# Third to eighth expert, last two tiles: two streams of one weight block joined into one of 512 columns, with VectorE adding the halves

## The reference, cut to what matters

```python
def _moe2_ref(x, w_gate, w_noise, noise, w1, w2):
    ...
    for e in range(E):                              # E = 8
        for k in range(2):
            mask = top2[:, k] == e
            h = np.maximum(x[mask] @ w1[e], 0.0)    # 512 -> 1024, the "up" product
            out[mask] += top2_w[mask, k, None] * (h @ w2[e])   # 1024 -> 512, "down"
```

## Time and profile before

| | us |
|---|---|
| median of three runs | 1014.07 (1013.69 to 1014.99) |
| the profiled execution | 1014.13 |
| its span, first to last instruction | 1012.3 |
| PE busy in it | 992.4 (98%) |
| DVE busy | 436.7 (43%) |
| ACT busy | 368.2 (36%) |
| POOL busy | 340.5 (34%) |

### The profile page before, as it was taken

How to read it: one execution, slowest core, us unless ns; L and a number is a source line. 1 busy time by engine, 2 the same in 40 slices (tenths; PEclk the granted TensorE clock), 3 DMA queues, 4 the chain that set the end, 5 groups by cost and what they waited for, 6 DMA issues and landing times. The chain is left out here.

```text
span 1012.3 us, 18602 instructions
## 1 busy us (share of the span) xinstructions
PE 992.4 (98%) x7173; PEld 903.5 (89%) x7173; DVE 436.7 (43%) x1188; ACT 368.2 (36%) x906; POOL 340.5 (34%) x317
## 2 busy tenths in 40 slices
PE   8999999999999999999999999999999999999994
PEld 7999898989989898999999898899998989898983
DVE  4664343442535345353355534443534434444410
ACT  5553343334324342432344423433434233343410
POOL 2780022121211212110112424563828373745211
PEclk9999999999999999999999999999999999999998
DMA  6655244242423324230234242772626465564312
GB/s 231 198 184 124 84 153 109 73 131 85 137 96 125 104 77 133 84 115 26 102 105 136 44 135 45 179 171 71 160 73 151 95 156 109 137 134 109 58 18 36
DMA packets 83098, 113.79 MB, mean 112 GB/s; under 512 B 19264, under 2 KB 45888, under 8 KB 83008
## 3 DMA queue, kind: packets, MB, share of 16 engines
q1 hardware_dynamic: 69104, 84.74, 27.8%
q0 software_dynamic: 13472, 27.31, 13.3%
q10 hardware_dynamic: 432, 0.52, 0.2%
HBM read 83.52 MB, written 29.02 MB: 111 GB/s over the span
## 5 line engine op out<-in xcount | busy, mean ns | idle before, releaser
L885 PEld LDWEIGHTS bank<-xr,wr 128*128 128x128 f32 x2592 | 325.0, 191 | 9.6 <-issue 0.8
L885 PE MATMUL bank<-xr,wr 128*128 128x256 f32 x2592 | 327.7, 283 | 0.4 <-issue 0.4
L986 PE MATMUL bank<-wr 128*128 128x256 f32 (+1 forms) x1536 | 229.3, 309 | 0.7 <-DVE xr L1554 0.4
L986 PEld LDWEIGHTS bank<-wr 128*128 128x128 f32 x1536 | 226.7, 190 | 2.2 <-DVE xr L1554 0.8
L707 POOL DMA_INDIRECT arena<-x_rows,shared x120 | 132.1, 1101 | 145.1 <-DVE v_nat L1542 96.8
L902 PE MATMUL bank<-wr,hr 128*128 128x512 f32 x648 | 174.9, 405 | 0.0
L1170 ACT ACTIVATE arena<-bank 128x256 f32<-128x256 f32 x108 | 41.4, 384 | 265.9 <-PE bank L885 257.0
L902 PEld LDWEIGHTS bank<-wr,hr 128*128 128x128 f32 x648 | 113.8, 188 | 26.9 <-issue 5.8
L1430 DVE SCALAR_TENSOR_TENSOR arena<-arena,bank 128x256 f32<-128x256 f32 x108 | 45.4, 420 | 211.6 <-ACT arena L1170 189.8
L1001 PE MATMUL bank<-wr 128*128 128x512 f32 x576 | 132.8, 390 | 0.0
L1001 PEld LDWEIGHTS bank<-wr 128*128 128x128 f32 x576 | 107.5, 188 | 21.9
(11 more groups left out here) (140 smaller groups left out, 739.9 us busy)
## 6 DMA issues: line engine op xcount, KB each, us to landing
arena<-moe_w SPq DMA_DIRECT2D x40, 512.0 KB
arena<-moe_w SPq DMA_DIRECT2D x96, 128.0 KB
p_rows<-arena SPq DMA_DIRECT2D x28, 256.0 KB, 2.1
v_nat<-p_rows SPq DMA_DIRECT2D x112, 64.0 KB
arena<-gv SPq DMA_DIRECT2D x12, 512.0 KB, 4.0
out<-zeros POOLq DMA_DIRECT2D x20, 256.0 KB, 3.2
x_rows<-arena SPq DMA_DIRECT2D x9, 512.0 KB, 4.3
arena<-v SPq DMA_DIRECT2D x34, 128.0 KB, 3.2
```

Source lines behind the costliest of these rows:

```text
L885: mm = pe.matmul(o, gv_w[:, f, w, kk], xr[:, g % 2, x, kk], start=(m + kk + n == 0), stop=(kk == KC - 1 and n == 2), skip_group_check=True)
L986: mm = pe.matmul(ps_h[u % 2][:, 0:n], w1_r[e % 2][:, a, kk, f * P:(f + 1) * P], xT[p][:, b, kk], start=(kk + x == 0), stop=(kk == KC - 1 a ...
```

## The change

For `p = 1` of experts 2 to 7 (`joint(e, p)`), a unit takes two matmuls for each `kk` in place of three. One has the high weights and streams the high and the low tokens one behind the other, 512 columns, into the two halves of the bank. The other has the low weights and streams the high tokens, 256 columns, into the first half. A new step on DVE, `add_hidden`, adds the two halves into `gate` with a `tensor_reduce` whose two inputs for each output lie 256 elements apart in the bank. `relu` and `hidden_low` of these units read `gate` instead of the bank. The new semaphore `hidden_added` tells ACT that the sum is there and PE that the bank is free; `joints(u)` counts the joined units up to `u`. Streamed columns of a unit stay as they were: 12 x 256 = 4 x 512 + 4 x 256 = 3072.

```diff
+        def joint(e, p):
+            return p == 1 and e >= AHEAD
+        def joints(u):
+            return sum(1 for i in range(u + 1) if i // F2C >= 2 * AHEAD and i // F2C % 2)
...
@@ up(e, p, f), on PE
-                if u >= 2:
+                if u >= 2 and joints(u - 2) > joints(u - 3):
+                    pe.wait_ge(hidden_added, joints(u - 2))
+                elif u >= 2:
                     pe.wait_ge(ht_lo, u - 1)
...
+                if joint(e, p):
+                    both = ps_h[u % 2].rearrange("p (a n) -> p a n", a=2)
+                    for kk in range(KC):
+                        pe.matmul(both, w1_r[e % 2][:, 0, kk, f * P:(f + 1) * P], xT[p][:, :, kk], start=(kk == 0), stop=False,
+                                  skip_group_check=True)
+                        mm = pe.matmul(both[:, 0], w1_r[e % 2][:, 1, kk, f * P:(f + 1) * P], xT[p][:, 0, kk], start=False,
+                                       stop=(kk == KC - 1), skip_group_check=True)
+                    mm.then_inc(up_done, 1)
+                    return
@@ relu(e, p, f), on ACT
+                if joint(e, p):
+                    act.wait_ge(hidden_added, joints(u))
+                    act.activation(hT[p][:, 0, f], gate[:, u % 2], ACT.Relu).then_inc(ht_hi, 1)
+                    return
@@ on DVE
+            def add_hidden(e, p, f):
+                u = F2C * half_no(e, p) + f
+                dve.wait_ge(up_done, u + 1)
+                dve.wait_ge(ht_lo, u - 1)
+                dve.tensor_reduce(gate[:, u % 2], ps_h[u % 2].rearrange("p (a n) -> p n a", a=2), AX.X, ALU.add
+                                  ).then_inc(hidden_added, 1)
...
@@ hidden_low(e, p, f)
+                if joint(e, p):
+                    dve.scalar_tensor_tensor(out=hT[p][:, 1, f], in0=gate[:, u % 2], scalar=0.0,
+                                             in1=hT[p][:, 0, f].bitcast(F32), op0=ALU.max, op1=ALU.subtract).then_inc(ht_lo, 1)
+                    return
```

More of the change, by code:

```diff
@@ L324, in attention_two_moe_program @@
         up_done = sem("up_done")
+        hidden_added = sem("hidden_added")
         ht_hi = sem("ht_hi")
@@ L1690, in _ @@
             for e in range(AHEAD, NE):
[L1691 to L1695, removed]
+                for f in range(F2C):
+                    hidden_low(e, 0, f)
+                    if f < KC:
+                        low(e, KC + f)
+                add_hidden(e, 1, 0)
+                for f in range(F2C):
+                    if f < F2C - 1:
+                        add_hidden(e, 1, f + 1)
+                    hidden_low(e, 1, f)
                 for a in range(TILES):
```

## The result

| | us |
|---|---|
| before, median of six runs | 1013.91 (1013.69 to 1014.99) |
| changed, median of six runs | 1019.25 (1017.47 to 1022.42) |
| ratio | 1.0052, 95% interval 1.0039 to 1.0065 |
| span of the profiled execution, before and after | 1012.3, 1018.2 |

The change is slower by half a per cent. 1011.5 us was forecast.

The account below looks back on a forecast made before the run. PE's matmul stream was taken to bound the kernel. Saving 53.3 ns in each of 48 units, 2.56 us, with nothing added by DVE or the later chain, gave 1011.5 us against 1014.07, range 1010.9 to 1014.3 us.

Parts of the forecast that it names:

- What bounds the kernel: Expert stretches of 55.40 us: PE busy throughout, so only the pace of its matmul stream counts.
- The fixed 13.3 ns for each matmul: Joined units: each matmul with weight load costs 13.3 ns beyond its columns; four fewer in each of 48 units save 2.56 us.
- rival (2): Joined units: the fixed 13.3 ns stays or switching widths costs as much, no gain, 1014.1 us; chance 0.13 with small gains.
- The reduction: DVE's `add_hidden`: reading 512 elements from the bank takes 0.69 us, whatever the distance between inputs.
- rival (1): DVE's `add_hidden`: far-apart inputs make the reduction slow, up to 1.22 us, PE waits, 1020.8 us; chance 0.12.
- The cover inside the joined part: Between joined units: PE's cover against waiting for the added halves grows from 0.40 to 0.50 us.
- The size of the delay: Behind the eighth unit: ACT's and DVE's work for the next expert starts 0.76 us later against PE.
- 384 matmuls fewer: Profile after the change: the count of matmuls was to fall by 384.
- the 2.5 ns: Skill page's gap for each warm matmul: by it only 0.5 us would go, giving 1013.6 us; the prediction followed the rows.
- What moves behind the units: Next expert's chain after the eighth unit: starting 0.76 us later costs nothing, with 6.7 us of room.
- Rival (3): Joined units: cover smaller than worked out, PE waits a little in some, 1012 to 1014 us; 0.05 with anything else.
- Slower: Outcome class for the whole kernel, slower than before: chance 0.14, from rival (1) and a remainder.

Follow-up runs that it names:

- b_late_084: Kernel before, plus a DVE operation of about 0.84 us ahead of the next expert's first transpose, experts 3 to 7, no joined matmuls: 1020.55 us, ratio 1.0057.
- a_unit_first: Changed kernel, with the fifth down tile and last tile's tokens handled on ACT and DVE only behind the next expert's first two up units: 1013.12 us, ratio 0.9986.
- b_late_short_low: Kernel before with the 0.84 us delay, and low parts of first-layer weight blocks of experts 4 to 8 cut to a quarter of their columns: 1014.65 us.
- a_short_low: Changed kernel, with low parts of first-layer weight blocks of experts 4 to 8 cut to a quarter of their columns: 1012.02 us, ratio 0.9977.

## Why the prediction was wrong, point by point

**Right.** What bounds the kernel: PE's stream. The fixed 13.3 ns for each matmul, in part: the joined parts shortened by 0.19 to 0.37 us where 0.43 was worked out, 1.50 us in place of 2.56 over the six. At 346 ns a pair the whole 13.3 ns that a pair was to save is gone; at 353 ns half of it is back, so rival (2) was half right in those parts. The reduction: 0.69 us forecast, 0.69 us measured, with inputs 256 elements apart in the bank, so rival (1) fell, and with it the worry that the rule of the Trainium skill ("SBUF — State Buffer", section "Door 1: The DMA port swizzle"), which is on matmuls, might hold for VectorE's reads of PSUM. The cover inside the joined part: no wait there in any trace. The size of the delay: "0.76 us later against PE"; the first transpose starts at 695.73 - 693.93 = 1.80 us after the first down matmul against 0.96 us before, so 0.84 us.

**Two slips that changed nothing.** "384 matmuls fewer" should be 192 (48 x 4; the profile's page counts 7173 before and 6981 after). And the 2.5 ns that the prediction takes from the section "Back-to-back issue gap" of the Trainium skill ("TensorE: Matmul & The Clock Gate") is given there for an isolated matmul, so it does not bear on a stream with weight loads like this one, whose 13.3 ns the rows give.

**The step that failed** is "What moves behind the units", with its "That costs nothing ... Cost nil, with 0.76 us of 6.7 us spent". It looked for the deadline of each moved piece at its own user: the third tile before the next p = 0 units (6.7 us of room), the last tile before the next p = 1 units (14 us). But the last tile has an earlier deadline that no user sets. In ACT's and DVE's queues the next expert's first `relu` and low part stand behind it, and PE needs these at its third unit. The row that gave the tile's end, 722.92 + 0.69 us, was read against 738.1 us; it had to be read against 725.62 us, less the `relu` and the low part that still have to follow. The cover there is 0.78 us. b_late_084 (the delay without the change costs 6.5 us) and a_unit_first (the late chain without that order costs nothing) show this step from both sides.

**A second miss in the same step** was to move the chain rigidly. The prediction names POOL's gathers among the late things, but gives them their old durations. Moved by 0.84 us, they fell over other DVE rows, took up to 0.77 us more each, and `rows_out` came 2.72 us later against PE. This miss was needed for the loss as well. In the kernel before ACT stands idle for 0.87 us ahead of that `relu`; with the last tile moved by 0.84 us and nothing lengthened, its low part would end at 722.92 + 0.69 + 0.84 = 724.45 us, 0.17 us after the moment at which the unit's low part starts now (724.28), and 0.6 us of the cover would be left. That is an estimate from these rows. It agrees with b_late_short_low and a_short_low, which show no break.

**A small miss**: the cover was worked out between joined units (0.50 us), not at the seam, where the second joined unit waits for a p = 0 unit's longer low part. It cost 0.055 us six times, 0.3 us in all.

Rival (3) named the right kind of event (PE waits a little in some units), at the wrong place and with far too small a price. "Slower" had a chance of 0.14, of which 0.12 was for rival (1), a mechanism that did not occur.

## What to carry to other kernels

When a change delays an in-order queue, look for what stands behind the delayed work in that queue, and take its deadline, not that of the delayed work's own user; the profile shows it as the row that follows, here the first `relu` of the next expert. A chain that passes through another engine's DMA instructions need not move rigidly, so a cover about as large as the delay is no cover. And where a gain on the bounding engine costs latency elsewhere, start the next chain earlier in the same edit: one moved transpose turned 1019.25 into 1012.86 us.

## What the runs showed of the hardware that was not expected

- POOL's indirect DMA instruction takes 0.95 us (gather of a quarter tile) or 1.6 us (scatter) alone, and up to 1.7 and 2.4 us where a DVE operation with two inputs in memory (128x1024, 1.18 us) runs beside it. With that operation cut to 256 columns the long ones at this place went away. Beside a shorter operation of that kind (128x512, 0.69 us) alone, 21 gathers of the kernel before took 0.94 to 0.99 us.
- A `tensor_reduce` on DVE that adds pairs 1024 bytes apart in PSUM reads 512 elements in 0.692 us, as long as a contiguous read of 512 elements (0.688 us).
- The pace of alternating 512- and 256-column matmuls has two steady values, 346 and 353 ns a pair, in one execution of one kernel. The cause is open.
